# A three-block transformer kernel: the second MLP by Strassen's seven block products, its hidden result kept in DRAM

## The reference

```python
mu = np.mean(x, axis=-1, keepdims=True)
var = np.mean((x - mu) ** 2, axis=-1, keepdims=True)
xn = (x - mu) / np.sqrt(var + 1e-06) * g_ln            # x: 4 x 576 x 512
ch = np.maximum(xn @ w_ch1, 0.0) @ w_ch2               # 512 x 2048, 2048 x 512
return x + ch
```

## Time and profile before

| | us |
|---|---|
| three runs | 714.2, 714.3, 715.52 |
| median | 714.3 |
| the profiled execution, its own time | 714.38 |
| its span (first to last instruction) | 712.6 |
| PE busy in the span | 701.6 (98%) |
| DVE, ACT, POOL busy | 323.9, 256.6, 199.8 |

### The profile page before, as it was taken

The page is one execution under the profiler, slowest core; times in us unless marked ns, Lnnn a source line. Parts: engine busy times, 40 slices in busy tenths (PEclk is TensorE's granted clock), DMA queues, the critical chain, the costliest instruction groups (busy, mean ns, idle before and its releaser), DMA issues.

```text
span 712.6 us, 12869 instructions
## 1 busy us (share of the span) xinstructions
PE 701.6 (98%) x4766; PEld 668.5 (94%) x4768; DVE 323.9 (45%) x1014; ACT 256.6 (36%) x756; POOL 199.8 (28%) x194
## 2 busy tenths in 40 slices
PE   8899999999999999999999999999999999999998
PEld 4579988999899989999999999999999999999998
DVE  6877973697469654834622142222223122312112
ACT  6755872487258534345311221212121112111110
POOL 1377233324333456453340211113020302010000
PEclk9999999999999999999999999999999999999999
DMA  8660006001500100133200001000100010001001
GB/s 292 225 227 1 1 14 214 1 3 35 192 0 0 60 1 1 65 120 137 94 21 25 1 1 45 1 0 1 45 1 1 0 45 1 1 1 46 0 1 45
DMA packets 15992, 35.02 MB, mean 49 GB/s; under 512 B 1728, under 2 KB 5696, under 8 KB 15936
## 3 DMA queue, kind: packets, MB, share of 16 engines
q1 hardware_dynamic: 15936, 34.29, 13.7%
HBM read 29.56 MB, written 4.72 MB: 48 GB/s over the span
## 4 chain that ended last, share of the span: by engine, by line
PE 97%; DVE 2%; issue 1%; POOL 0%; ACT 0%; DVEq 0%; ACTq 0%; POOLq 0%
PE bank L952 29%; PE bank L954 29%; PE bank L953 29%; PE bank L976 3%; PE bank L1005 3%; PE bank L989 3%; DVE probs L736 1%; PE bank L960 1%; PE bank L1068 1%; PE bank L1069 1%; DVE probs L749 0%; DVE res L923 0%; PE bank L1075 0%; PE bank L1074 0%; DVE win_hi L724 0%
## 5 line engine op out<-in xcount | busy, mean ns | idle before, releaser
L915 DVE SCALAR_TENSOR_TENSOR hid_lo<-bank,hid_hi 128x384 fp32r<-128x384 f32 x96 | 53.5, 558 | 280.7 <-ACT hid_hi L678 280.7
L678 ACT ACTIVATE hid_hi<-bank 128x384 fp32r<-128x384 f32 x96 | 47.1, 491 | 300.4 <-PE bank L954 300.4
L953 PE MATMUL bank<-xn_lo,w_hi 128*128 128x384 f32 x384 | 129.5, 337 | 0.0
L954 PE MATMUL bank<-hid_hi,w_lo 128*128 128x384 f32 x384 | 129.5, 337 | 0.0
L952 PE MATMUL bank<-hid_hi,w_hi 128*128 128x384 f32 x384 | 129.4, 337 | 0.0
L954 PE MATMUL bank<-xn_hi,w_lo 128*128 128x384 f32 x384 | 129.2, 336 | 0.0
L952 PE MATMUL bank<-xn_hi,w_hi 128*128 128x384 f32 x384 | 129.0, 336 | 0.0
L953 PE MATMUL bank<-hid_lo,w_hi 128*128 128x384 f32 x384 | 128.9, 336 | 0.0
L539 ACT ACTIVATE probs<-probs,stat 96x128 f32<-96x128 f32 (+2 forms) x192 | 71.8, 376 | 14.2 <-DVE stat L736 14.0
L952 PEld LDWEIGHTS bank<-hid_hi,w_hi 128*128 128x128 f32 x384 | 72.2, 188 | 0.0
L954 PEld LDWEIGHTS bank<-xn_hi,w_lo 128*128 128x128 f32 x384 | 72.1, 188 | 0.0
(11 more groups left out here) (97 smaller groups left out, 1303.9 us busy)
## 6 DMA issues: line engine op xcount, KB each, us to landing
w_raw<-w_ff_dram SPq DMA_DIRECT2D x16, 512.0 KB, 3.5
v_sb<-vW_dram SPq DMA_DIRECT2D x16, 384.0 KB, 6.4
k_sb<-kT_dram SPq DMA_DIRECT2D x15, 304.0 KB, 6.4
q_sb<-qT_dram SPq DMA_DIRECT2D x15, 288.0 KB, 6.1
out_dram<-res SPq DMA_DIRECT2D x5, 768.0 KB, 3.8
res<-w_sgT_dram SPq DMA_DIRECT2D x1, 1152.0 KB, 10.7
win_v_raw<-w_in_dram SPq DMA_DIRECT2D x4, 256.0 KB, 6.7
win_u_raw<-w_in_dram SPq DMA_DIRECT2D x4, 256.0 KB, 8.3
```

What stands on the lines that cost most here:

```text
L678: act.activation(hid_hi[:, f % 2, :], h_bank[f % 2][:, 0:TILE], ACT.Relu).then_inc(hh_ready, 1)
L915: dve.scalar_tensor_tensor(out=hid_lo[:, f % 2, :], in0=h_bank[f % 2][:, 0:TILE], scalar=0.0, in1=hid_hi[:, f % 2, :].bitcast(F32), op0=AL ...
L953: pe.matmul(dst, wh, xl, start=False, stop=False)
L954: last = pe.matmul(dst, wl, xh, start=False, stop=(stop and i == n - 1))
```

## The change

Both products of the second MLP are made by Strassen's scheme in its form with fewer additions: each matrix is seen as 2 x 2 blocks, and seven products of sums of blocks (P1, P2, P6, P7, P5, P3, P4 in PE's order) take the place of eight. A tile is now a batch: two token halves of 288 columns by two feature halves. First the hidden matrix of all four batches is made, a pair of weight units ("lockstep") at a time; a product fills a pair of banks (two times 288 columns), DVE combines products in `stage`, ACT rectifies, and SP stores to DRAM. Then the second matrix is made batch by batch from quarters read back into `res`. The four sums of weights (S) and of activations (T) are formed on POOL; every block or sum is rounded on ACT into one of seven slots of `xf_hi`, and its rest made on DVE or POOL into `xf_lo`. The residual x goes to DRAM too (`save_x`) and comes back for the last addition. There are 4 x 4 x 7 x 12 hidden matmuls and 4 x 7 x 4 x 12 output matmuls, all of 288 columns. The layer norm is by halves of 288; batches 0 and 1 are normalised inside phase A (in period 1 and in the last period), 2 and 3 in tiles 1 and 2.

The core of the diff:

```diff
-EARLY = 3
-DVE_W2 = (0, 1, 2, 8, 9)
+EARLY = 4
+
+
+FORMS = 7
+P1, P2, P6, P7, P5, P3, P4 = range(FORMS)
+W_AT = (0, 1, 3, 4, 5, 6, 2)
+W_PLAIN = (P1, P2, P4)
...
+
+
+def statistics_after(n, q, i):
+    place = {(0, P6): 0, (0, P5): 1, (1, P1): 2, (1, P6): 3}.get((q, i))
+    return None if place is None or n + 1 not in LATE_NORMS else 4 * (n + 1) + place
+
...
+
+            def load_unit(g):
+                if g >= 2:
+                    sp.wait_ge(plain_lo, g - 1)
...
+            def sum_weights(g):
+
+                u = g % UNITS
+                a11, a12, a22, a21 = (w_raw[:, g % 2, i * BLOCK:(i + 1) * BLOCK] for i in range(4))
+                s1, s2, s3, s4 = (sum_at(u, i) for i in (P5, P6, P7, P3))
+                pool.wait_ge(wff_in[g % 2], 16 * (g // 2 + 1))
+                wait_unit(pool, g)
+                pool.tensor_tensor(s1, a21, a22, ALU.add).then_inc(w_sum, 1)
+                pool.tensor_tensor(s3, a11, a21, ALU.subtract).then_inc(w_sum, 1)
+                pool.wait_ge(w_sum, 4 * g + 1)
+                pool.tensor_tensor(s2, s1, a11, ALU.subtract).then_inc(w_sum, 1)
+                pool.wait_ge(w_sum, 4 * g + 3)
+                pool.tensor_tensor(s4, a12, s2, ALU.subtract).then_inc(w_sum, 1)
...
+            def form_t2(e):
+                pool.wait_ge(xl_dve, fills_by(False, fill_of(e, P1)))
+                pool.wait_ge(t3_done, e + 1)
+                pool.tensor_tensor(quarter_at(e, 0), quarter_at(e, 1), quarter_at(e, 0),
+                                   ALU.add).then_inc(t2_done, 1)
+
+            def form_t1(e):
+                wait_slot(pool, fill_of(e, P5))
+                pool.wait_ge(t2_done, e + 1)
+                pool.tensor_tensor(form_source(fill_of(e, P5)), quarter_at(e, 3), quarter_at(e, 0),
+                                   ALU.subtract).then_inc(t1_done, 1)
+
+            def form_t4(e):
+                wait_slot(pool, fill_of(e, P4))
+                wait_quarter(pool, e, 2)
+                pool.wait_ge(t2_done, e + 1)
+                pool.tensor_tensor(form_source(fill_of(e, P4)), quarter_at(e, 2), quarter_at(e, 0),
...
             def last_period(b):
                 pool.wait_ge(pv_ready, B * TWINS)
-                pool.memset(xc[:, 0:P], 1.0 / DM).then_inc(b_const, 1)
-                pool.memset(eps_c[:], EPS).then_inc(b_const, 1)
-                pool.wait_ge(b_const, 2)
-                pool.tensor_copy(mean_w[:], xc[:, 0:P]).then_inc(b_const, 1)
-                pool.wait_ge(res_done, NOUT + 1)
-                sum_x(0)
-                split_sum(0, False)
+                statistic(4)
+                statistic(5)
+                sum_weights(0)
+                statistic(6)
+                statistic(7)
                 split_all_v(b)
-                sum_squares(0)
-                split_sum(0, True)
+                split_plain(0)
+                sum_weights(1)
                 for i in range(NMIX):
                     split_gated(b, i)
-                split_xn(0, 0)
+                    if i == 0:
+                        split_plain(1)
+                    if i == 1:
+                        sum_weights(2)
+                    if i == 3:
+                        split_plain(2)
+                    if i == 4:
+                        form_t3(0)
+                form_t2(0)
+                split_form(fill_of(0, P7))
+                form_t1(0)
+                split_form(fill_of(0, P3))
+                form_t4(0)
+                for g in range(3, EARLY):
+                    sum_weights(g)
+                    split_plain(g)
...
+            def hidden_tile(n):
+                if n + 1 in LATE_NORMS:
+                    for i in range(4):
+                        statistic(4 * (n + 1) + i)
...
+                                split_plain(g)
+                        if q == 3:
+                            form_t3(n + 1)
+                            form_t2(n + 1)
+                            split_form(fill_of(n + 1, P7))
+                            form_t1(n + 1)
+                            split_form(fill_of(n + 1, P3))
+                            form_t4(n + 1)
+                    else:
+                        if q == 0:
+                            for j in range(PIECES):
+                                form_t3(B + j)
+                        else:
+                            for g in (UNITS + 2 * q - 2, UNITS + 2 * q - 1):
+                                sum_weights(g)
+                                split_plain(g)
+
+            def output_step(s):
+                g = (B + 1) * FORMS + s
+                if g >= FORMS * SETS:
+                    return
+                e, i = set_of(g), form_of(g)
+                if i == P2 and e >= B + PIECES:
+                    form_t3(e)
+                elif i == P6:
+                    form_t2(e)
+                elif i == P5:
+                    form_t1(e)
+                elif i == P4:
...
+            for s in range(B * STEPS2):
+                if s == 0:
+                    split_plain(2 * UNITS - 2)
+                    split_plain(2 * UNITS - 1)
+                if s == 3:
+                    sum_weights(2 * UNITS - 2)
+                if s == 5:
+                    sum_weights(2 * UNITS - 1)
...
             def gelus(b, first=False, last=False):
+                if b == 1:
+                    act.wait_ge(b_const, 3)
+                    sum_hi(0)
+                    sum_hi(1)
+                    squares(0, 0)
                 if last:
-                    act.wait_ge(b_const, 3)
-                    sum_hi(0, False)
+                    sum_hi(4)
+                    plain_high(0)
+                    sum_hi(5)
+                    squares(1, 0)
+                    sums_high(0)
                 if first:
                     for s in range(NS):
                         split_wsg(s)
                 for s in range(NS):
                     gelu_v(b, s)
-                    if last and s == 1:
-                        norm_squares(0, (0, 1))
+                    if (last or b == 1) and s == 1:
+                        n = 1 if last else 0
+                        sum_hi(4 * n + 2)
+                        squares(n, 1)
+                    if (last or b == 1) and s == NS - 1:
...
+                if units:
+                    plain_high(g)
+                rectify(m, P2, 0)
+                if norm and q == 0:
+                    sum_hi(4 * (n + 1) + 1)
+                    squares(n + 1, 0)
...
+                if units:
+                    sums_high(g)
+                if q == 3:
+                    form_high(following)
+                    form_high(following + 1)
+                rectify(m, P5, 3)
+                if norm and q == 0:
+                    sum_hi(4 * (n + 1) + 2)
+                    squares(n + 1, 1)
...
+                if units:
+                    plain_high(g + 1)
+                if q == 3:
+                    form_high(following + 2)
+                rectify(m, P3, 1)
+                if q == 3:
+                    form_high(following + 3)
+                rectify(m, P4, 2)
...
+                if units:
+                    sums_high(g + 1)
+                if q == 3:
+                    form_high(following + 4)
+                    form_high(following + 5)
+                    form_high(following + 6)
...
+            plain_high(2 * UNITS - 2)
+            plain_high(2 * UNITS - 1)
+            for s in range(B * STEPS2):
+                g = (B + 1) * FORMS + s
+                if s % STEPS2 == PIECES - 1:
+                    copy_p1(B * LOCKSTEPS + s // STEPS2)
+                if g < FORMS * SETS:
+                    form_high(g)
+                if s == 5:
+                    sums_high(2 * UNITS - 2)
+                if s == 8:
+                    sums_high(2 * UNITS - 1)
 
...
+            def combine(m, i, dst, src):
+
+                wait_product(dve, m, i)
+                wait_past(dve, drained, m * FORMS + (DRAINED[i - 1] if i > P2 else 0))
+                if dst is None:
+                    n = m - B * LOCKSTEPS
+                    dve.wait_ge(y_added, 4 * n + Y_ADDED[P7])
+                    to, x = output_at(src), output_at(src)
+                else:
+                    to, x = stage[:, :, dst, :], stage[:, :, src, :]
+                dve.tensor_tensor(to, product_at(m, i), x, ALU.add).then_inc(drained, 1)
...
+            for s in range(B * STEPS2):
+                if s % PIECES == PIECES - 1:
+                    output_product(s // STEPS2, s % STEPS2 // PIECES)
+                g = (B + 1) * FORMS + s
+                if g < FORMS * SETS and not by_pool(g):
+                    split_form(g)
+                if s == 6:
+                    split_sums(2 * UNITS - 2)
+                if s == 9:
+                    split_sums(2 * UNITS - 1)
 
...
+                for x, (lo, col) in enumerate(first):
```

(39 more changed lines are left out.)

928 lines of the change are left out of this document (623 added, 305 removed).

## The result

The changed kernel takes 806.9 us (median of four runs, 804.5 to 807.7) against 714.3 in the same session: a ratio of 1.129, interval 1.126 to 1.132. The prediction said 753 and a range of 720 to 780. The direction was right, the size was not: 93 us lost where 39 were forecast. The profiled execution has a span of 802.4 us, against 712.6 before.

What follows compares the result with a forecast made beforehand. PE's columns were taken to bound the kernel, at full clock. From 714.4 us: minus 44.9 for columns, plus waits and clock of 6.4, 12.5, 0.5, 31, 18, 8 and 7, gave 753; range 720 to 780.

Steps and rivals of the forecast that it cites:

- Part 1: Second MLP's columns: fewer, narrower matmuls at 0.133 us each, and a shorter end; with phase A's norm columns, minus 44.9 us.
- Part 2: Norm in phase A: PE waits behind POOL's and ACT's queues, 6.4 us in period 1 and 12.5 in the last.
- Part 3: Hidden-tile borders: PE waits for helper chains; 31 us over tiles 1 to 3 (13, 13, 5), 0.5 at tile 0.
- Part 4: Crossing to the second matrix: PE waits 6.6 and 11.3 us for late weight units; sum 18 us.
- Part 5: SBUF port in the second matrix: DVE's splits and POOL's operations exclude each other; 8 us, between 0 and 18.
- Part 6: PE's clock: stretches at 1.2 GHz after waits of 2.5 us or more; 7 us, between 0 and 14.
- 3: Rival: the port binds the second matrix, 0.2 us lost at each of 48 handovers, batch 57 to 60; 778 us, chance 0.12.
- 4: Rival: clock stays low over long parts, half clock for a fifth of the second matrix, 18 more; 771 us, chance 0.08.
- 1: Rival: helpers keep ahead at the tile borders and in phase A, so waits shrink; 692 us, chance 0.13.
- 2: Rival: the waits are there but shorter, since pieces put in a row overlap; 722 us, chance 0.12.

Runs made afterwards that it cites:

- kernel 9: Changed kernel with the squares of batch 1's norm behind the Gelus and POOL's splits of v in phase A's last period: 807.0 us, ratio 1.129.
- kernel 12: On top of kernel 8 and kernel 9, DVE instead of POOL splits the gated values, and scales batch 1 in tile 0: 743.2 us, ratio 1.038.
- Kernel 6: Changed kernel with DVE's split of unit 15's weight sums ahead of the first T1 form's split instead of behind it: 802.1 us, ratio 1.124.
- kernel 5: Changed kernel with POOL's four additions of x each standing four steps later in POOL's order, work unchanged: 794.8 us, ratio 1.112.
- Kernel 1: Changed kernel with spare PE matmuls meant for its six longest waits, of which four were filled: 805.1 us, ratio 1.126.
- kernel 8: Changed kernel with norm, T3 sums, unit 15's split, P1's copy and fourth-sum rounding reordered, additions of x on DVE: 749.7 us, ratio 1.049.

## Why the prediction was wrong

**Part 1, the columns:** right in the price, 2688 matmuls at 0.133 us; phase B's columns and the norm's are 359 us of 469. But the phase before ends at 709.65, not at the 708.1 that I read from the chain's piece, so 47.0 us of columns were saved, not 45.4; and from PE's last product to the end of the span it is 3.9 us instead of 2.9, one more where I had 0.9 less.

**Part 2, phase A:** forecast 20.3 with columns, measured 26.6: the last period took 70.5 us instead of 54.7, period 1 80.1 instead of 70.2. The waits named are there (4.0 and 3.0 for statistics, 1.9 for the Gelus), but it isn't only the order that I followed: with another order the same time was lost behind it (kernel 9), and with work taken from POOL 3.0 us of phase A came back (kernel 12). That POOL's time is short fits both; where the rest of the 26.6 goes stays open.

**Part 3, the borders:** the waits of 8.1 and 8.0 us at the norm's first product were forecast as 8.2. The fourth product waited 4.4 and 3.0, forecast 3.2. With a last one of 1.9 in tile 2 the waits are 12.5 and 12.9, as forecast; matmuls at 1.2 GHz and what is left over make 16.8 and 17.1 of them. And tile 3, forecast 5, took 16.1: P1's copy 4.6 (forecast 4.0), and the 6.3 us chain behind POOL's T3 sums, which waited 17.0 for a load. I listed T3's cost, not what it would wait for at the head of its queue.

**Part 4, the crossing:** forecast 18, measured 25.4 with what the clock took; the two waits were 10.7 and 4.5 where I had 11.3 and 6.6, and a third of 2.8 for a form's split was missed. Kernel 6 shows that such waits aren't worth their length: 8.4 us of wait gone, 3.4 us gained.

**Part 5 is the step that failed.** "I take 8, near the middle of 0 and 18", for the port, and the three later batches lost 29.6: 22 of the 51 us by which the forecast is short in the trace (tile 3 is the next, 11). The port was priced nearly right: 48.5 against 44.8 us a batch, by the rows above, 11 us for three. What I left out is that the four additions of x, which stand in "20 + 4 POOL operations" as work alone, each wait for a finished block with the next batch's sums queued behind them: 13 us by kernel 5. I also let the lead of seven slots absorb 8 us (and by my own sum, 9 to 18 less 8, the term would have been 1 to 10, not 0 to 18); that it absorbs nothing once POOL's stops have used it up fits the rows but no run shows it. I asked what is queued behind each wait of PE, and not behind each wait of POOL.

**Part 6, the clock:** forecast 7. The low stretches were many more than I counted (78 us), and my first reading put a large part of the loss on them: at half speed for the 51 us in which PE was busy, 25 at most. Kernel 1 speaks against that for the stages that it filled. By the Trainium skill (TensorE: Matmul & The Clock Gate, "What's actually happening") activity releases the throttle; the trace agrees, since filling the waits removed 30 us of low clock. It did not follow that time was to be had. For the three later batches the clock's share stays open.

**The rivals:** 3 had the right place and a batch of 57 to 60 (measured 55.6), by handovers that cost 0.2; the cause was half another, and that the rest is the port was not shown by an edit of its own. 4 had the stretches right (38 us of low clock in the second matrix, 36 forecast), but not their price of 18: in the first batch, where two waits were filled, they cost nothing; in the others it wasn't tried. 1 and 2 are excluded by the result. That kernel 8 comes near the forecast of 753 bears nothing out, as it is a kernel in another order; and even it isn't faster than the kernel before. The range was too narrow upwards, since it took each unknown term at its middle and gave no term for what I had not found.
